# The first two attention units and the first MLP block of a fused kernel, reordered

## The reference

```python
def _attn_ref(q, k, v, mem_k, mem_v):            # q, k, v: (4, 8, 768, 64), 8 memory keys
    chunk, left_ctx, right_ctx = (32, 16, 8)
    for c in range(S // chunk):
        k_full = concat(mem_k, k[l_start:r_end]); v_full = concat(mem_v, v[l_start:r_end])
        scores = scale * q_c @ k_full.T
        scores = scores - max(scores); a = exp(scores)
        a = a / (sum(a) + 1e-09)
        out[chunk] = a @ v_full
def _moe_ref(x, w_in, w_out):                    # x: (3072, 512), w_in: (512, 2048)
    h = x @ w_in
    return (h * (1.0 / (1.0 + exp(-h)))) @ w_out
def _moe2_ref(x, phi, w1, w2):                   # 32 slots, 8 experts
    logits = x @ phi
    d = softmax(logits, 0); slot_input = d.T @ x
    slot_out[e] = relu(slot_input[e] @ w1[e]) @ w2[e]
    return softmax(logits, 1) @ slot_out
```

## Time and profile before

| | us |
|---|---|
| median of the runs | 475.18 |
| the profiled execution | 476.51 |
| its span in the profile | 474.7 |
| PE busy | 453.1 (95%) |
| DVE / ACT / POOL busy | 275.1 / 138.7 / 45.3 |
| first MLP matmul starts at | 19.16 |
| first MLP matmul of block 1 starts at | 62.14 |

### The profile page before, as it was taken

One profiled execution on the slowest core, in us unless ns is written; L12 is line 12 of the kernel. 1 busy time (PEld: TensorE's weight loads), 2 busy tenths in 40 slices (PEclk: granted clock), 3 DMA queues, 4 the chain that ended last, 5 costly groups with the idle time before them and its releaser, 6 DMA issues.

```text
span 474.7 us, 12275 instructions
## 1 busy us (share of the span) xinstructions
PE 453.1 (95%) x5460; PEld 333.7 (70%) x5460; DVE 275.1 (58%) x531; ACT 138.7 (29%) x255; POOL 45.3 (10%) x43
## 2 busy tenths in 40 slices
PE   5899999999999999999999999999999999999972
PEld 5799667777776787767777677777677879634541
DVE  5657458665596566766666676558444556532123
ACT  2655233232331333323233323233111312201012
POOL 2475000000000000000000000000000000100000
PEclk9999999999999999999999999999999999999987
DMA  8989222220221122302221122020260489999996
GB/s 334 419 307 387 76 97 101 102 90 18 94 101 48 55 101 101 101 1 101 102 100 44 59 101 91 12 89 1 99 257 1 179 338 420 420 384 423 420 412 285
DMA packets 14308, 81.59 MB, mean 172 GB/s; under 512 B 1584, under 2 KB 1712, under 8 KB 7856
## 3 DMA queue, kind: packets, MB, share of 16 engines
q1 hardware_dynamic: 14256, 80.81, 43.8%
HBM read 74.51 MB, written 6.29 MB: 170 GB/s over the span
## 4 chain that ended last, share of the span: by engine, by line
PE 85%; DMA 6%; DVE 4%; ACT 1%; POOL 1%; issue 1%; DVEq 0%; SPq 0%; POOLq 0%
PE h_ps L294 54%; PE o_ps L276 6%; DMA unit<-w 5%; PE lpu_ps L310 5%; PE lpu_ps L330 4%; PE sx_ps L253 3%; PE pt_ps L262 2%; PE sx_ps L330 2%; PE h_ps L948 1%; PE sx_ps L885 1%; POOL sc L763 1%; PE lpu_ps L318 1%; PE h_ps L885 1%; DMA qk_sb<-qk 1%; PE o_ps L928 1%
## 5 line engine op out<-in xcount | busy, mean ns | idle before, releaser
L294 PE MATMUL h_ps<-x_odd,wh 128*128 128x512 f32 x384 | 126.8, 400 | 0.0
L499 DVE SCALAR_TENSOR_TENSOR gT<-gT,h_ps 128x512 f32<-128x512 f32 (+1 forms) x108 | 66.5, 616 | 98.1 <-ACT gT L398 97.6
L398 ACT ACTIVATE gT<-h_ps 128x512 f32<-128x512 f32 (+1 forms) x108 | 58.6, 543 | 185.5 <-PE h_ps L294 184.4
L294 PEld LDWEIGHTS h_ps<-x_odd,wh 128*128 128x128 f32 x384 | 72.1, 188 | 21.4 <-issue 5.1
L294 PE MATMUL h_ps<-x_even,wh 128*128 128x512 f32 x256 | 85.0, 400 | 0.0
L294 PE MATMUL h_ps<-x_odd,wl 128*128 128x512 f32 x192 | 74.9, 390 | 0.0
L509 DVE STREAM_TRANSPOSE gB<-gT 128x512 f32<-128x512 f32 x80 | 56.7, 709 | 1.9
L294 PEld LDWEIGHTS h_ps<-x_even,wh 128*128 128x128 f32 x256 | 48.0, 188 | 12.6 <-issue 2.2
L763 POOL TENSOR_TENSOR sc<-sc,row_stats 128x512 f32<-128x512 f32 x24 | 25.1, 1045 | 280.7 <-DVE row_stats L483 280.7
L294 PE MATMUL h_ps<-x_short,wh 128*128 128x256 f32 x256 | 50.6, 290 | 0.3 <-DVE x_short L488 0.3
L294 PE MATMUL h_ps<-x_even,wl 128*128 128x512 f32 x128 | 49.9, 390 | 0.0
(11 more groups left out here) (167 smaller groups left out, 494.4 us busy)
## 6 DMA issues: line engine op xcount, KB each, us to landing
unit<-w SPq DMA_DIRECT2D x32, 1024.0 KB, 10.6
qk_sb<-qk SPq DMA_DIRECT2D x24, 640.0 KB, 4.1
v_sb<-v SPq DMA_DIRECT2D x24, 512.0 KB, 5.5
out<-unit SPq DMA_DIRECT2D x6, 1024.0 KB, 7.7
w_stage<-w_in SPq DMA_DIRECT2D x4, 1024.0 KB, 11.0
wot<-w_outT SPq DMA_DIRECT2D x4, 1024.0 KB, 11.7
unit<-w_out SPq DMA_DIRECT2D x4, 1024.0 KB, 6.5
part<-phi SPq DMA_DIRECT2D x1, 64.0 KB, 3.9
```

Source lines behind the costliest of these rows:

```text
L294: last = nc.tensor.matmul(h_ps[k % 2][:, 0:TOKS[b]], w[:, n, kc, q * 128:(q + 1) * 128], x[:, lo, kc, 0:TOKS[b]], start=(kc == 0 and w is ...
L398: nc.scalar.activation(gt_of(b, k), h_ps[k % 2][:, 0:TOKS[b]], ACT.Tanh, scale=0.5).then_inc(tanh_done, 1)
L499: nc.vector.scalar_tensor_tensor(out=gt_of(b, k), in0=gt_of(b, k), scalar=1.0, in1=h_ps[k % 2][:, 0:TOKS[b]], op0=ALU.add, op1=ALU.mult).t ...
```

## The change

Seven edits, all in the beginning and in block 0:

1. The transfer of q and k of unit 0 is split into two, by pairs of heads (the layout in memory is changed to match). Scores of unit 0 are made in two halves of 16 matmuls; DVE takes the maxima by halves (`dve_first_scores`).
2. DVE and POOL each do half of the multiplication by the inverse for units 0 and 1 (`normalise`).
3. Unit 1 has its own `pt_second` and uses the bank `lp_ps` for its values, so that it doesn't wait for unit 0 to give back `pt` and `o_ps`.
4. The low part of half 1 of w_in goes from DVE to POOL (`W_LOW_BEFORE`), and the first MLP step of each column group now waits for both halves.
5. The first w_in transfer is issued ahead of v of unit 0. ACT and DVE have their work of the beginning in another order.
6. In block 0 the scores of the next unit come before the values of the current one, on PE, DVE and ACT.
7. `pe_w2` goes from after step 13 to after step 9, `pe_w2_T` from after step 14 to after step 10, with DVE's part of both.

```diff
-W_LOW_BEFORE = {2: (0,), 3: (2, 3), 4: (4, 5), 5: (6, 7)}
+W_LOW_BEFORE = {1: (0,), 2: (1,), 3: (2, 3), 4: (4, 5), 5: (6, 7)}
...
+        pt_second = at("pt_second", R + 7 * HALF_W, [128, 4 * PAIRS, QT])
...
         def pe_scores(pe, u, dispatched=0):
-            pe.wait_ge(qk_in[u % QK_RING], 16 * (u // QK_RING + 1))
+            if u == 0:
+                pe.wait_ge(qk_first, 16)
+            else:
+                pe.wait_ge(qk_in[u % QK_RING], 16 * (u // QK_RING + 1))
...
+            for ps in (range(0, 2), range(2, 4)) if u == 0 else (range(PAIRS),):
+                if u == 0 and ps[0]:
+                    last.then_inc(s_first, 1)
+                    pe.wait_ge(qk_in[0], 16)
...
         def pe_probs_T(pe, u):
             pe.wait_ge(p_done, u + 1)
+            if u < 2:
+                pe.wait_ge(p_half, u + 1)
...
         def pe_values(pe, u):
-            if u:
+            if u == 1:
+                pe.wait_ge(sc_done, 2)
+            elif u:
                 pe.wait_ge(x_done, u)
...
         def pe_mlp(pe, b, k):
             if b == 0 and q == 0:
-                if n == 0:
-                    pe.wait_ge(wl_first, 1)
-                pe.wait_ge(wl_done, 2 * n + 1)
+                pe.wait_ge(wl_done, 2 * n + 2)
...
+                if b == 0 and at_pause:
+                    pe_scores(pe, scores_at(0, n))
                 if at_pause and values_at(b, n) is not None:
                     pe_values(pe, values_at(b, n))
...
-                if b == 0 and k == 13:
+                if b == 0 and k == 9:
                     pe_w2(pe)
-                if at_pause and scores_at(b, n) is not None:
+                if b and at_pause and scores_at(b, n) is not None:
                     pe_scores(pe, scores_at(b, n), b if k > dispatch_step(b) else 0)
-                if b == 0 and k == 14:
+                if b == 0 and k == 10:
                     pe_w2_T(pe)
...
+        def dve_first_scores(dve):
+
+            maxima = rmax[:, 0, :].rearrange("p (a g) -> p a g", a=2)
+            for a, scored in enumerate((s_first, s_mm)):
+                dve.wait_ge(scored, 1)
+                nc.vector.memset(sx_ps[:, a, 0:LEFT], NEG).then_inc(edge_first, 1)
+                dve.wait_ge(edge_first, a + 1)
+                nc.vector.tensor_reduce(maxima[:, a, :], by_window(0)[:, a, :, :], AX.X, ALU.max).then_inc(max_first, 1)
+            dve.wait_ge(max_first, 2)
+            nc.vector.tensor_tensor(sc_of(0), by_window(0), maxima.unsqueeze(3).to_broadcast([128, 2, 4, WIN]),
+                                    ALU.subtract).then_inc(sc_done, 1)
...
+        def normalise(ops, eng, u, lo, hi, done):
+
+            eng.wait_ge(rinv_done, u + 1)
+            p = sc[:, u % SB, lo:hi, :]
+            ops.tensor_tensor(p, p, rinv[:, u % SB, lo:hi].unsqueeze(2).to_broadcast([128, hi - lo, WIN]),
+                              ALU.mult).then_inc(done, 1)
...
-            load_qk(0)
+            sp.dma_start(qk_sb[:, 0, :, 0:QKW // 2], qk[0, :, :, 0:QKW // 2]).then_inc(qk_first, 16)
+            sp.dma_start(qk_sb[:, 0, :, QKW // 2:QKW], qk[0, :, :, QKW // 2:QKW]).then_inc(qk_in[0], 16)
             load_qk(1)
+            load_w_in(0)
             load_v(0)
-            load_w_in(0)
             load_v(1)
...
             nc.vector.memset(pt[:], 0.0).then_inc(pt_zero, 1)
-            dve_scores(dve, 0)
-            dve_scores(dve, 1)
-            dve_sums(dve, 0)
-            dve_sums(dve, 1)
-            pt_half(dve, nc.vector.tensor_copy, 0, 1)
+            nc.vector.memset(pt_second[:], 0.0).then_inc(pt_zero, 1)
             nc.vector.memset(negmax[:, 1:2], -NEG)
             nc.vector.memset(total[:], 0.0)
+            dve_first_scores(dve)
+            dve_sums(dve, 0)
+            normalise(nc.vector, dve, 0, 4, 2 * PAIRS, p_half)
+            dve_scores(dve, 1)
+            pt_half(dve, nc.vector.tensor_copy, 0, 1)
+            dve_sums(dve, 1)
+            normalise(nc.vector, dve, 1, 4, 2 * PAIRS, p_half)
+            pt_half(dve, nc.vector.tensor_copy, 1, 1)
             dve_x(dve, 0)
-            pt_half(dve, nc.vector.tensor_copy, 1, 1)
-            low_part(nc.vector, dve, 1, wl_first)
             dve_x(dve, 1)
```

More of the change, by code:

```diff
@@ L1 @@
+import itertools
 from contextlib import ExitStack
@@ L234, in sc_of, with pt_of, o_of @@
             return sc[:, u % SB, :, :].rearrange("p (a g) k -> p a g k", a=2)
+        def pt_of(u):
+            return pt_second if u == 1 else pt
+        def o_of(u):
+            return lp_ps if u == 1 else o_ps
         def heads(ap):
@@ L246, in pe_scores @@
                 pe.wait_ge(acc_done, 4 * dispatched - 1)
-            for t in range(2):
-                for c in range(2):
-                    for p in range(PAIRS):
-                        for h2 in range(2):
-                            a, r = place_of(p, h2)
-                            at = (2 * t + c) * WIN
-                            last = nc.tensor.matmul(s_of(u)[32 * r:32 * r + 32, a, at:at + WIN], q_of(u, t, c, p, h2),
-                                                    k_of(u, t, c, p, h2), start=True, stop=True)
+            for ps in (range(0, 2), range(2, 4)) if u == 0 else (range(PAIRS),):
+                if u == 0 and ps[0]:
+                    last.then_inc(s_first, 1)
+                    pe.wait_ge(qk_in[0], 16)
+                for t, c, p, h2 in itertools.product(range(2), range(2), ps, range(2)):
+                    a, r = place_of(p, h2)
+                    at = (2 * t + c) * WIN
+                    last = nc.tensor.matmul(s_of(u)[32 * r:32 * r + 32, a, at:at + WIN], q_of(u, t, c, p, h2),
+                                            k_of(u, t, c, p, h2), start=True, stop=True)
             last.then_inc(s_mm, 1)
@@ L275, in pe_values @@
                         at, h = p * UT + t * QT, 2 * p + h2
-                        last = nc.tensor.matmul(o_ps[64 * h2:64 * h2 + 64, at:at + QT],
-                                                v_sb[:, u % V_RING, t, h * D:(h + 1) * D], pt[:, (2 * a + t) * 4 + r, :],
+                        last = nc.tensor.matmul(o_of(u)[64 * h2:64 * h2 + 64, at:at + QT],
+                                                v_sb[:, u % V_RING, t, h * D:(h + 1) * D], pt_of(u)[:, (2 * a + t) * 4 + r, :],
                                                 start=True, stop=True)
@@ L402, in pt_half @@
             eng.wait_ge(p_tr, u + 1)
-            if u:
+            if u < 2:
+                eng.wait_ge(pt_zero, u + 1)
+            else:
                 eng.wait_ge(o_mm, u)
-            else:
-                eng.wait_ge(pt_zero, 1)
             half = slice(64 * c, 64 * c + 64)
-            copy(pt[half, :, c * CHUNK:(c + 1) * CHUNK],
+            copy(pt_of(u)[half, :, c * CHUNK:(c + 1) * CHUNK],
                  pt_ps[half, :].rearrange("p (j q) -> p j q", q=CHUNK)).then_inc(pt_done, 1)
@@ L427, in act_x @@
             act.wait_ge(o_mm, u + 1)
-            nc.scalar.copy(hi, heads(o_ps)).then_inc(xh_done, 1)
+            nc.scalar.copy(hi, heads(o_of(u))).then_inc(xh_done, 1)
         def act_dispatch(act, b):
@@ L455, in act_block @@
                     act_dispatch(act, b - 1)
-                if k % 4 == pause(b) + (b == 0) and scores_at(b, n) is not None:
+                if at_pause and scores_at(b, n) is not None:
                     act_exp(act, scores_at(b, n))
+        def dve_first_scores(dve):
[8 more added lines that the diff above has]
+                                    ALU.subtract).then_inc(sc_done, 1)
         def dve_scores(dve, u):
@@ L468, in dve_scores @@
             if first or last:
-                dve.wait_ge(edge_done, 2 * (u // BATCH_UNITS) + 1 + last)
+                dve.wait_ge(edge_done, 2 * (u // BATCH_UNITS) + last)
             nc.vector.tensor_reduce(rmax[:, u % SB, :].rearrange("p (a g) -> p a g", a=2), by_window(u), AX.X, ALU.max).then_inc(max_done, 1)
-            dve.wait_ge(max_done, u + 1)
+            dve.wait_ge(max_done, u)
             nc.vector.tensor_tensor(sc_of(u), by_window(u),
@@ L487, in dve_x @@
             dve.wait_ge(xh_done, u + 1)
[L488 removed]
+            nc.vector.tensor_tensor(lo, heads(o_of(u)), hi.bitcast(fp32), ALU.subtract).then_inc(x_done, 1)
         def low_part(ops, eng, m, done):
@@ L566, in dve_block @@
                 n, at_pause = k // 4, k % 4 == pause(b)
-                if b and k % 4 == pause(b) + 1 and scores_at(b, n) is not None:
+                if k % 4 == pause(b) + 1 and scores_at(b, n) is not None:
                     dve_sums(dve, scores_at(b, n))
@@ L573, in dve_block @@
                 dve_g(dve, b, k)
-                if b == 0 and k % 4 == pause(b) + 1:
-                    dve_sums(dve, scores_at(b, n))
+                if b == 0 and at_pause:
+                    dve_scores(dve, scores_at(0, n))
                 if at_pause and values_at(b, n) is not None:
@@ L770, in _ @@
             act_exp(act, 0)
+            act_wh(act, 0)
+            act_pt(act, 0)
             act_exp(act, 1)
```

(4 more changed lines are left out.)

17 lines of the change are left out of this document (8 added, 9 removed).

## The result

The changed kernel takes 479.78 us (median of five runs, 479.03 to 480.97) where the kernel before takes 475.09 beside it; the ratio is 1.0089 (95% interval 1.0071 to 1.0108). It is 4.7 us slower: the forecast was 474.6, its range ended at 476.5.

What follows compares the result with a forecast made beforehand. PE, always busy from 62 to 380 us, was taken as the bound, so only an earlier block 1 could help. Head -1.2, waits -1.6 and product +2.2 gave -0.6 us: 474.6 us, range 473.0 to 476.5.

Steps and rivals of the forecast that it cites:

- The head: Up to the first MLP matmul: starts 1.2 us earlier, at about 18.0 instead of 19.16; bounds 0 to 1.45.
- The split transfer adds 0.1 to 0.2.: Load queue: rows of 1280 instead of 5120 bytes make the last part of `wot` land 0.1 to 0.2 us later.
- The rival on the head: Head: halves in turn and slow small rows leave a gain of 0.3 us, sum +0.3, 475.5 us; chance 0.10.
- The passes move by 0.1 only: Head, PE: 20 warm-up passes of 2.50 us move by 0.1, so unit 0's transposes start at 10.3, not 11.75.
- POOL's half in 0.65 us: Head, unit 1: POOL's half of the multiplication runs from 13.2 to 13.85, transposes at 13.9; bounds 0.52 and 1.04.
- The lock that the forecast left in a sentence beside: Head: DVE and POOL share an exclusive port, making POOL's half of unit 1 0.4 us later, head gain 0.8.
- The waits of block 0: Block 0: old waits for POOL and w2c go, 2.8 us, against 1.2 of new ones; net gain 1.6 us.
- The new waits for the gating: Block 0: PE waits three times for DVE's gating of hidden activations, 1.2 us in all; bounds 0 and 1.8.
- The product: Block 0, w_out and phi after step 9: PE stands 2.2 us for the last part of `wot`; 1.2 to 4.5.
- the working of the landing: Load queue: the last part of `wot` lands at 42.8; 41.8 at the full rate, 45.1 at the pace of before.
- The clock: Product in block 0: PE's clock falls after its wait, remaining work 1.6 us longer, +1.0, 476.2 us; chance 0.11.
- The forecast's own sign of being wrong: Product in block 0: forecast is wrong if PE has no wait for `wot`, or one of over 3 us.

Runs made afterwards that it cites:

- e4: Kernel before with only the transfer of q and k of unit 0 split in two, scores waiting for both: 478.04 us, ratio 1.0065.
- e1: Changed kernel with q and k of unit 0 in one transfer again, its scores and maxima whole: 476.61 us, ratio 1.0033 to before.
- e2: Changed kernel with the product of w_out and phi back after step 13, its transpose after step 14: 475.31 us, ratio 1.0001 to before.
- e16: The changed kernel unchanged, measured once more: 479.66 us, ratio 1.0087 to the kernel before.
- e5: Changed kernel with one whole transfer, scores and maxima for unit 0, and the product back behind steps 13 and 14: 472.94 us, ratio 0.9953 to before.
- e11: e5 with VectorE alone multiplying unit 1 by the inverses, GpSimd nothing: 476.28 us, ratio 1.0008 to before.
- e12: e5 with exp of unit 1 ahead of unit 0's copy, 12 warm-up passes for 20, VectorE alone multiplying unit 1: 471.90 us, ratio 0.9917 to before.
- Experiment 1: Four kernels, one edit each: e1, e2 and e3 against the changed kernel, e4 against the kernel before; 476.61, 475.31, 479.84 and 478.04 us.
- e3: Changed kernel with v of unit 0 issued ahead of the first w_in transfer, as before: 479.84 us, ratio 1.0096 to before.

## Why the prediction was wrong, by its own steps

**The head (forecast -1.2, measured +2.9): this step failed**, in three pieces that come to 4.0 of the 4.1 between 17.96 and 22.04.

- *"The split transfer adds 0.1 to 0.2."* I priced it by its short rows and gave it to `wot` only. Its cost is on the next transfer in the queue: q and k of unit 1, whose scores moved from 6.95 to 9.38, 2.4 us. I had treated unit 1's scores as unaffected. The rival on the head named "a slow start of the small rows", with 475.5 as its time; the place was nearly right, the small rows were not the cause, and its 0.9 us stand against 2.7 to 3.2 for the split alone (e4, e1).
- *"The passes move by 0.1 only", with 2.50 us from the earlier trace rows.* They took 3.78: 1.3 us, by their pace from a low clock. This piece was a draw and not a price of the change: with the same head they take 2.50 in e2 and 4.09 in e16, and without the wait 3.21 in e5 and 2.50 in e11, whose code is the same up to there. So 2.50 in the earlier trace rows was one draw too. With the same head as the changed kernel, e2's first MLP matmul is at 20.34 and e16's at 22.49: the head lost 1.2 to 3.3 us, never gained. With 2.50 the transposes stand at 10.47 (e11), where I had 10.3.
- *POOL's half in 0.65 us.* From transposes to transposes the units are 3.90 apart, 3.6 forecast: 0.3. Of these, 0.2 are POOL's half, 0.85 and not 0.65. The lock that the forecast left in a sentence beside is what e11 and e12 show, and it should have been in the sum.

**The waits of block 0 (forecast -1.6, measured -2.0): right in mechanism, two terms too large.** All went, and block 0 is 2.04 us shorter in e2 and e5. The new waits for the gating, 1.2 in the forecast, are 0.2 at the most; the 0.15 that I added to each old wait was not there either, since the four rows as printed add up to 2.17. That the net came near is partly luck: 0.6 too much on one side, 1.0 on the other.

**The product (forecast +2.2, measured +3.9).** In e1, whose head gave 0.3 and not 1.2 and whose waits gave more than I had counted, the product starts at 40.69 and the last part is there at 43.25, against 40.0 and 42.8 forecast; block 0 is 2.67 us longer than e5's (43.61 and 40.94). So the working of the landing holds; its bound of 45.1 was not reached. One step of it fails: it counted the standing from the fourth matmul, 40.6, while what is lost counts from the start of the product (Experiment 1). From 40.0 the forecast's own landing gives 2.8 and not 2.2. In the changed kernel PE comes 3.2 later (43.89) and the part 4.4 later (47.68), and 3.2 of these have a reason: the transfer ahead of it in the list is released by PE's own scores, and it is issued at 29.22, in e1 at 26.01. The other 1.2 are open. What delays PE delays the load as well, so lateness in the head did not make the wait shorter. By the time, the place of the product costs 4.5 us in the changed kernel (e2) and 3.7 between e1 and e5.

**The clock.** The rival had it falling while PE stands for `wot`. Nothing shows that: from 47.6 to 51.2 the column reads 1.00, and the 26 matmuls behind the wait take 3.62 us in the changed kernel, in e1, e3 and e16 alike. What the forecast never asked about was the head, where the passes' time moves by up to 1.6 us between executions of the same head.

**The sum.** -1.2 - 1.6 + 2.2 = -0.6; measured +2.88 - 2.04 + 3.88 = +4.72. The forecast's own sign of being wrong, standing of over 3 us for `wot`, came true as well: 3.7 by the starts of the groups.
